# Windowed attention inside a two-layer feed-forward kernel: the probabilities of the loop are normalised and turned by VectorE in 32x32 blocks instead of by TensorE, the heads are turned straight out of PSUM, and the values run three steps after their scores

## What is computed

```python
scores = scale * np.matmul(q_c, k_full.transpose(0, 1, 3, 2))      # 32 queries x 64 keys
scores = scores - np.max(scores, axis=-1, keepdims=True)
a = np.exp(scores)
a = a / (np.sum(a, axis=-1, keepdims=True) + 1e-09)
out[:, :, c_start:c_end] = np.matmul(a, v_full)
...
h = x @ w_in;  g = np.maximum(0.01 * h, h);  x = g @ w_out          # first block, 512 -> 2048 -> 512
...
h = x @ w_in2; g = P(h) / (Q(h) + 1e-6);     y = g @ w_out2         # second block, the same sizes
```

## Time and profile before

| | |
|---|---|
| median of 3 runs | 1153.5 us (1151.1 to 1154.75) |
| profiled execution, its own time | 1152.93 us |
| its span in the trace | 1151.1 us |
| PE busy | 1136.9 us, 99% |
| VectorE busy | 741.6 us, 64% |
| ScalarE busy | 565.9 us, 49% |
| GpSimd busy | 132.6 us, 12% |
| granted TensorE clock, mean | 0.997 of full speed |

### The profile page before, as it was taken

How to read it: one execution, slowest core, us unless ns; L and a number is a source line. 1 busy time by engine, 2 the same in 40 slices (tenths; PEclk the granted TensorE clock), 3 DMA queues, 4 the chain that set the end, 5 groups by cost and what they waited for, 6 DMA issues and landing times.

```text
span 1151.1 us, 22841 instructions
## 1 busy us (share of the span) xinstructions
PE 1136.9 (99%) x8950; PEld 1066.0 (93%) x8950; DVE 741.6 (64%) x1385; ACT 565.9 (49%) x1184; POOL 132.6 (12%) x132
## 2 busy tenths in 40 slices
PE   7999999999999999999999999999999999999998
PEld 6999999999999999999999999999999999999996
DVE  5554444444445454443327888888888888888886
ACT  4223223323233332322227676676767667676765
POOL 4991120211202112100000000000000000000000
PEclk8999999999999999999999999999999999999999
DMA  7662434334434255210786010020201002020000
GB/s 265 198 201 102 169 108 156 130 114 157 163 131 154 74 184 175 83 56 2 285 278 241 1 65 18 1 83 1 83 1 71 13 1 83 1 83 1 28 1 28
DMA packets 44311, 114.77 MB, mean 100 GB/s; under 512 B 5040, under 2 KB 5168, under 8 KB 44208
## 3 DMA queue, kind: packets, MB, share of 16 engines
q1 hardware_dynamic: 44208, 113.33, 28.5%
HBM read 77.66 MB, written 35.65 MB: 98 GB/s over the span
## 4 chain that ended last, share of the span: by engine, by line
PE 95%; DVE 2%; ACT 1%; issue 1%; DMA 0%; SPq 0%; DVEq 0%
PE psum L512 15%; PE psum L514 15%; PE psum L513 15%; PE psum L527 8%; PE psum L546 8%; PE psum L547 8%; PE psum L545 8%; PE psum L528 7%; PE psum L529 7%; PE psum L484 2%; PE psum L461 1%; PE psum L469 1%; DVE g_lo L860 1%; DVE scratch L857 0%; ACT g_hi L688 0%
## 5 line engine op out<-in xcount | busy, mean ns | idle before, releaser
L512 PE MATMUL psum<-x_hi,w_hi 128*128 128x384 f32 x1020 | 342.5, 336 | 1.5 <-DVE x_lo L851 1.5
L514 PE MATMUL psum<-x_hi,w_lo 128*128 128x384 f32 x1020 | 342.6, 336 | 0.0
L513 PE MATMUL psum<-x_lo,w_hi 128*128 128x384 f32 x1020 | 341.6, 335 | 0.0
L857 DVE TENSOR_TENSOR scratch<-psum,scratch 128x384 f32<-128x384 f32 x128 | 71.3, 557 | 237.6 <-ACT scratch L682 236.9
L682 ACT ACTIVATE scratch<-psum 128x384 f32<-128x384 f32 x128 | 62.8, 491 | 279.2 <-PE psum L514 275.3
L512 PEld LDWEIGHTS psum<-x_hi,w_hi 128*128 128x128 f32 x1020 | 191.5, 188 | 8.4 <-issue 2.3
L513 PEld LDWEIGHTS psum<-x_lo,w_hi 128*128 128x128 f32 x1020 | 191.5, 188 | 5.4
L514 PEld LDWEIGHTS psum<-x_hi,w_lo 128*128 128x128 f32 x1020 | 191.4, 188 | 0.0
L527 PE MATMUL psum<-g_hi,w_hi 128*128 128x384 f32 x512 | 177.5, 347 | 0.0
L529 PE MATMUL psum<-g_hi,w_lo 128*128 128x384 f32 x512 | 171.3, 335 | 0.0
L528 PE MATMUL psum<-g_lo,w_hi 128*128 128x384 f32 x512 | 171.2, 334 | 0.0
(11 more groups left out here) (75 smaller groups left out, 1407.4 us busy)
## 6 DMA issues: line engine op xcount, KB each, us to landing
raw<-weights_in SPq DMA_DIRECT2D x64, 256.0 KB, 4.1
scratch<-groups_in SPq DMA_DIRECT2D x21, 768.0 KB, 6.1
scratch<-groups_in SPq DMA_DIRECT2D x21, 512.0 KB, 4.4
w_hi_scratch<-w_high SPq DMA_DIRECT2D x32, 256.0 KB, 4.1
w_lo_scratch<-raw SPq DMA_DIRECT2D x32, 256.0 KB, 4.5
w_hi<-w_hi_scratch SPq DMA_DIRECT2D x32, 256.0 KB, 3.6
w_lo<-w_lo_scratch SPq DMA_DIRECT2D x32, 256.0 KB, 4.5
x_hi_scratch<-x_hi SPq DMA_DIRECT2D x8, 768.0 KB, 3.3
```

The source lines that it names most:

```text
L512: nc.tensor.matmul(bank, hi, x_hi[:, b, k, :], start=(k == 0), stop=False)
L513: nc.tensor.matmul(bank, hi, x_lo[:, b, k, :], start=False, stop=False)
L514: last = nc.tensor.matmul(bank, lo, x_hi[:, b, k, :], start=False, stop=(k == KT - 1))
```

## The change

Only the 21 groups inside the loop change; the first three keep the old functions under new names (`scores_first`, `values_first`, `save_first_heads`, and `first_maxima` with the exponential `first_exp`, which two of them had already).

In the loop the subtraction of the maximum goes into the bias of the exponential, which becomes eight activations of 64 columns, each with its row sum as a second output. DVE then inverts the sums, multiplies all probabilities by them, and turns them with eight transposes, each on 32 partitions by 256 columns. PE's four transposes, ACT's copy and DVE's sum of the rows go. The products of the values run after `gemm1` of the third step after their scores, not the second; DVE turns their result from PSUM directly and saves it in that same step. PE waits with the next scores for `turned`, no longer for `x_ready`. The order of the 32 products within the scores and within the values changes too, and with it the layout of `q`, `k` and `v` in the input, of the same size.

```diff
-TRANSPOSE_AT = {f + 1: g for f, g in SCORES_AT.items()}
-VALUES_AT = {f + 2: g for f, g in SCORES_AT.items()}
-SAVE_AT = {f + 3: g for f, g in SCORES_AT.items()}
+TURN_AT = {f + 1: g for f, g in SCORES_AT.items()}
+VALUES_AT = {f + 3: g for f, g in SCORES_AT.items()}
...
                 if not own_place:
-                    pe.wait_ge(x_ready, g)
+                    pe.wait_ge(turned, g)
...
             def scores(c, at):
+
+                for cc in range(CPG):
+                    for u in range(2):
+                        for q in range(SLOTS):
+                            st, j = q // 2, 2 * u + q % 2
+                            last = nc.tensor.matmul(
+                                psum[CHUNK * q:CHUNK * (q + 1), at.bank + u, KEYS * cc:KEYS * (cc + 1)],
+                                q_of(ring(c), st, j, cc), k_of(ring(c), st, j, cc), start=True, stop=True)
...
+                if own_place:
+                    pe.wait_ge(probs_t_ready, g + 1)
+                else:
+                    pe.wait_ge(probs_turned, g - GPT + 1)
 
             def values(c, at):
+
+                for cc in range(CPG):
+                    for j in range(SLOTS):
+                        for st in range(SETS):
+                            q0 = (j % 2) * 2 * P + (j // 2 * CPG + cc) * CHUNK
+                            last = nc.tensor.matmul(
+                                at.loop_values_at[CHUNK * j:CHUNK * (j + 1), st, :, cc, :],
+                                at.probs_t[DH * st:DH * (st + 1), q0:q0 + CHUNK],
+                                v_of(ring(c), st, j, cc), start=True, stop=True)
...
-                        if f in TRANSPOSE_AT:
-                            transpose_probs(g0 + TRANSPOSE_AT[f], loop_att[TRANSPOSE_AT[f]])
...
+            def loop_exp(g, at):
+
+                act.wait_ge(shifted, g + 1)
+                for u in range(2):
+                    for c in range(CPG):
+                        n = CPG * u + c
+                        last = nc.scalar.activation(at.loop_probs[:, n, :], at.scores[:, u, c, :], ACT.Exp,
+                                                    scale=SCALE, bias=at.safe[:, n:n + 1],
+                                                    accum_out=at.loop_sums[:, n:n + 1])
+                last.then_inc(exp_ready, 1)
...
+            def turn_probs(g, at):
+
+                dve.wait_ge(exp_ready, g + 1)
+                nc.vector.tensor_scalar(at.safe, at.loop_sums, SUM_EPS, None, ALU.add).then_inc(sums_ready, 2)
+                dve.wait_ge(sums_ready, 3 * g + 2)
+                nc.vector.reciprocal(at.loop_inv, at.safe).then_inc(sums_ready, 1)
+                dve.wait_ge(sums_ready, 3 * g + 3)
+                nc.vector.tensor_tensor(at.loop_probs, at.loop_probs,
+                                        at.loop_inv.unsqueeze(2).broadcast_to([P, SETS * CPG, KEYS]),
+                                        ALU.mult).then_inc(normalised, 1)
+                dve.wait_ge(normalised, g + 1)
+                for q in range(SLOTS):
+                    for h in range(2):
+                        to = CHUNK * (q // 2 * 2 + h)
+                        last = nc.vector.transpose(
+                            at.probs_t[to:to + CHUNK, (q % 2) * 2 * P:(q % 2 + 1) * 2 * P].rearrange("p (n k) -> p n k", k=CHUNK),
+                            at.loop_halves[CHUNK * q:CHUNK * (q + 1), :, h, :])
+                last.then_inc(probs_turned, 1)
+
+            def turn_values(g, at):
+
+                dve.wait_ge(heads_ready, g + 1)
+                nc.vector.transpose(at.probs_t.rearrange("p (s n) -> p s n", s=SETS), at.loop_values).then_inc(turned, 1)
```

More of the change, by code:

```diff
@@ L161, in build @@
     probs_t_ready = S("probs_t_ready")
+    probs_turned = S("probs_turned")
     heads_ready = S("heads_ready")
@@ L224, in __init__ @@
             self.heads_tv = probs_t.rearrange("p (e k n) -> p e k n", e=2, k=KT)
+            self.loop_probs = probs.rearrange("p (n k) -> p n k", k=KEYS)
+            self.loop_halves = probs.rearrange("p (n h k) -> p n h k", h=2, k=CHUNK)
+            self.loop_values = psum[:, bank:bank + 2, 0:2 * SETS * DH]
+            self.loop_values_at = self.loop_values.rearrange("p s (h c r) -> p s h c r", h=DHALVES, r=CHUNK)
+            self.loop_heads = probs_t.rearrange("p (k n) -> p k n", k=KT)
+            self.loop_sums = st[:, 1, :]
+            self.loop_inv = st[:, 3, :]
             self.max_v = st[:, 0, :].rearrange("p (s c) -> p s c", s=SETS)
@@ L486, in values @@
                                     at.probs_t[DH * c2:DH * (c2 + 1), q0:q0 + CHUNK],
-                                    v_of(ring(c), st, j, cp, c2), start=True, stop=True)
+                                    first_v_of(ring(c), st, j, cp, c2), start=True, stop=True)
                 last.then_inc(heads_ready, 1)
@@ L613, in first_scores @@
                 wait_scores(g, g, own_place=True)
-                scores(g, first_att[g])
+                scores_first(g, first_att[g])
             def first_values(g):
-                wait_values(g, g)
-                values(g, first_att[g])
+                wait_values(g, g, own_place=True)
+                values_first(g, first_att[g])
             pe.wait_ge(zeros_ready, 1)
@@ L669, in save_probs_t, with save_heads, save_first_heads @@
                 nc.scalar.copy(at.probs_t, psum[:, at.bank, :]).then_inc(probs_t_ready, 1)
-            def save_heads(g, gi, b, at, t=None):
+            def save_heads(g, gi, b, at, t):
                 act.wait_ge(turned, g + 1)
-                if t is not None and gi == 0:
+                if gi == 0:
                     act.wait_ge(y_stored, 32 * t + 1)
+                nc.scalar.copy(x_hi[:, b, :, P * gi:P * (gi + 1)], at.loop_heads).then_inc(xh_ready, 1)
+            def save_first_heads(g, gi, b, at):
+                act.wait_ge(turned, g + 1)
                 to = x_hi[:, b, :, P * gi:P * (gi + 1)].rearrange("p k (e n) -> p e k n", e=2)
@@ L742, in tile_a @@
                         if f in SCORES_AT:
[L743 to L747, removed]
+                            loop_exp(g0 + SCORES_AT[f], loop_att[SCORES_AT[f]])
+                        if f in VALUES_AT:
+                            save_heads(g0 + VALUES_AT[f], VALUES_AT[f], (tp + 1) % 2, loop_att[VALUES_AT[f]], t)
                 save_y_high(t, tp)
@@ L813, in first_maxima, with loop_maxima, save_low @@
                 nc.vector.tensor_scalar(at.safe, at.st[:, 0, :], -SCALE, None, ALU.mult).then_inc(shifted, 1)
+            def loop_maxima(g, gi, tp, t, at):
+                dve.wait_ge(scores_ready, g + 1)
+                edge = None
+                if tp == 0 and gi == 0:
+                    edge = at.scores[:, :, 0, N_MEM:N_MEM + LEFT]
+                if tp == 1 and gi == GPT - 1:
+                    edge = at.scores[:, :, CPG - 1, KEYS - RIGHT:KEYS]
+                if edge is not None:
+                    nc.vector.tensor_scalar(edge, edge, NEG, None, ALU.add).then_inc(masked, 1)
+                    dve.wait_ge(masked, t + 1)
+                first_maxima(g, at)
+            def turn_probs(g, at):
[18 more added lines that the diff above has]
+                nc.vector.transpose(at.probs_t.rearrange("p (s n) -> p s n", s=SETS), at.loop_values).then_inc(turned, 1)
+            def save_low(g, gi, b, at):
+                dve.wait_ge(xh_ready, g + 1)
+                cols = slice(P * gi, P * (gi + 1))
+                nc.vector.tensor_tensor(x_lo[:, b, :, cols], at.loop_heads, x_hi[:, b, :, cols].bitcast(F32),
+                                        ALU.subtract).then_inc(x_ready, 1)
             def first_inverses(g, at):
@@ L1002, in windows @@
         return full.reshape(BATCH, HEADS, n_groups, CPG, KEYS, DH)
-    slots = np.array([[SLOTS * (p // 2) + 2 * (p % 2) + (r + p // 2) % 2 for r in range(2)] for p in range(HEADS // 2)])
+    slots = np.array([[SLOTS * (p // 2) + 2 * ((r + p // 2) % 2) + p % 2 for r in range(2)] for p in range(HEADS // 2)])
     qg = q.reshape(BATCH, HEADS, n_groups, P, DH)[:, slots].transpose(0, 3, 2, 5, 1, 4)
     kg = windows(k, mem_k)[:, slots].transpose(0, 3, 2, 6, 1, 4, 5)
-    vg = windows(v, mem_v).reshape(BATCH, SETS, SLOTS, n_groups, 2, 2, KEYS, DH).transpose(0, 3, 4, 6, 1, 5, 2, 7)
+    vw = windows(v, mem_v).reshape(BATCH, SETS, SLOTS, n_groups, CPG, KEYS, DH)
+    vg = vw.transpose(0, 3, 1, 5, 4, 2, 6).reshape(GROUPS, P, -1)
+    first_vg = vw.reshape(BATCH, SETS, SLOTS, n_groups, 2, 2, KEYS, DH).transpose(0, 3, 4, 6, 1, 5, 2, 7).reshape(GROUPS, P, -1)
+    vg = np.concatenate([first_vg[:GPT], vg[GPT:]])
     groups = np.concatenate([a.reshape(GROUPS, P, -1) for a in (qg, kg, vg)], axis=2)
```

36 lines of the change are left out of this document (20 added, 16 removed).

## The result

The changed kernel takes 1156.39 us (median of 20 runs, 1154.13 to 1159.04) against 1152.94 for the kernel before (20 runs): ratio 1.0032, 95% interval 1.0024 to 1.0041. The forecast was 1145.3 us with a range from 1141 to 1156. It was wrong, and in its sign. The profiled execution of the changed kernel has a span of 1153.6 us where the one before had 1151.1. Of the later experiments, one run of e1 (3978.97 us) and one of e3 (1840.88 us) were slow ones, and their ratios go without them.

A forecast was written before the change was run, and what follows sets the result against it. TensorE, busy 99% of the span, was taken to bound the kernel. Removing 13.1 us of transposes and waits, less 3.4 and 1.5 us of POOL stalls, gave 8.2 us gain: 1145.3 us, range 1141 to 1156.

The forecast's parts named there:

- What goes: On PE: 21 groups' transposes (9.3 us), their waits for the exponential (1.6) and for x_lo (2.2) disappear, 13.1 us together.
- the waits for `x_lo`: PE before the scores: three stalls from DVE's late x_lo, 2.2 us together, vanish because PE waits for turned instead.
- the sum: PE time removed by the change: 9.3 + 1.6 + 2.2 = 13.1 us, before stalls are taken off.
- What moves at no cost: PE's products of scores and values: new order taken as free, 0.99 us each; a price could make 4 us either way.
- SP's delay of one step: SP's load of v and the weights' stores and loads come one step later, with 61 us of cover.
- The new chain: On DVE and ACT, from H (end of the gemm1 before the maxima): probs_turned at 193.75, 0.1 us before PE's deadline.
- The choice between 2.9 and 3.8 us for the turning: DVE's eight transposes per group: 2.9 us if they overlap (rival, chance 0.24), 3.8 us if not; the upper taken.
- The spare: Between the end of the DVE and ACT chain and PE's deadline before the values: 0.1 us left.
- POOL's surcharge: PE stalls from DVE instructions reading two SBUF tiles beside POOL: 3.4 us in the first tile, 1.5 us later.
- The dear transposes: Rival: DVE's transposes cost more, PE waits for probs_turned in all 21 groups; 1165.9 us at 0.60 each; slower, chance 0.13.
- in most groups: Sign that the forecast is wrong: PE stands before the values in most groups.
- The forecast's own number: Whole kernel: 13.1 - 3.4 - 1.5 = 8.2 us faster, 1145.3 us; chance 0.40.

The follow-up runs named there:

- e1: Changed kernel with the loop groups' row maxima in PSUM, read there by the scaling: 1150.28 us, 0.9984 of the kernel before.
- e3: Changed kernel with POOL's splits of the second block's weights cut to 8 of 512 columns: 1151.09 us, 0.9990 of the kernel before.
- e10: Kernel before without the loop's transposes on PE and ACT's copy behind them: 1141.66 against 1153.17 us, 0.9903.
- e7: e2 with the hidden tile also kept in PSUM: 1140.52 us, 0.9882 of the kernel before; second go 1142.32 us, 0.9908.
- e9: Kernel before with only the hidden tile kept in PSUM between the maximum and g_lo: 1150.71 against 1153.17 us, 0.9982.
- e5: Changed kernel with neighbouring DVE transposes on the same 32 partitions, one execution: the eight take 3.09 us in place of 3.59.
- e2: e1 with epsilon's output and the inverses also in PSUM: 1143.3 against 1151.63 us for the kernel before, 0.9930.
- c0: Changed kernel again with no edit, on a second chip: 1157.38 against 1153.32 us for the kernel before, 1.0038.
- e8: e1 without adding epsilon, the reciprocal made directly from the sums: 1145.55 us, 0.9924 of the kernel before.

## Why the prediction was wrong

**What goes** was right. The transposes and their waits were put at 10.9 us, and e10 measured 11.2 us (9.2 to 13.0). With the waits for `x_lo` the sum was 13.1 us; e7, in which no stall is left before the values, gains 13.6 and 10.6 us in two goes. It removes the same waits for the exponential and for `x_lo` as e9, so the two gains don't add. No wait for `x_lo` before the scores stands in the trace after.

**What moves at no cost** was right. Scores and values still take 0.99 us each in their new order, and SP's delay of one step cost nothing visible.

**The new chain** was right: H + 12.36 measured for H + 12.47. The choice between 2.9 and 3.8 us for the turning fell on the right side, measured 3.59, and e5 shows why the upper one holds. The spare was 0.3 us rather than 0.1.

**The step that failed is POOL's surcharge.** It was put at 3.4 + 1.5 = 4.9 us and measured 13.8 us of stalls (8.3 + 5.5), with 1.6 us at the lower clock behind them. Its list had three instructions that wait for POOL, those that read two tiles from SBUF. It left out the two small ones that the change puts into the chain, the scaling of the maxima (L865) and the epsilon (L883). They read one tile and write eight columns, I priced them at 0.17 us, and each takes up to 1.25 us when POOL is at work. For the later groups I looked at `g_lo` alone and found it at the edges of POOL's work; L865 starts 1.2 us after it, between these edges, and met POOL in seven groups. There it made the 5.5 us, as e1 and e3 show from both sides. In the first tile it is four or five waits in a row. By their durations less the undisturbed ones, L865 waited 2.3 us in the three groups, L883 2.6, `g_lo` 2.1 and the multiplication 1.1. So the three instructions that I had priced waited 3.2 us, about the 3.4 that I gave them (after the spare), and the two that I had left out waited 4.9 us; together they made stalls of 8.3 us.

The kernel before had the warning in it. Its own small instruction on such columns, L828, has a median of 172 ns and a longest of 548, by the source view of that line:

```profile
L828 DVE TENSOR_SCALAR stats<-stats x22: 170/172/548, 10.2 to 524.1; 128x8 f32<-128x8 f32 x22
```

I had taken its duration from a clean group. The Trainium skill states the mechanism too (SBUF — State Buffer, Who interferes with whom): `tensor_scalar` may use the port pair that DVE shares with POOL, which is held by one of them for a whole instruction, and `tensor_reduce` never does. The runs agree: `tensor_scalar` took 1.24 us beside POOL from SBUF and 0.166 always from PSUM (e1), and the `tensor_reduce` of the kernel before that reads SBUF (L826) took at most 0.682 us, beside POOL too. No transpose in the 168 of the changed kernel was over 0.442 us either.

**The clock** was in no term. After a stall of 3.9 us in the first group PE ran 3.4 us at half its clock and lost 1.6 us more.

**Of the rivals** none named what happened. The dear transposes had the right wait and the wrong cause; that PE stands before the values "in most groups" did not come true either (10 of 21). The gain was there; it was given back to a wait of an instruction that I had counted as nothing.

**Luck.** The forecast's own number, 8.2 us faster, is near what e2 measures, 8.1 us, but by chance: e2 takes the multiplication out of POOL's way as well and has 2.0 us of stalls left where the forecast had 4.9, so the sum would give it 11.1. The traces show where the rest went. Ahead of the loop the granted clock is at half for a time that differs from one execution to the next (6.8 us in the kernel before and in the changed kernel, 13.7 in c0's execution of the same kernel and in e2's), and the loop's first scores start at 30.39 us in the kernel before and at 31.94 in e2. Counted from these scores to the end, the kernel before takes 1120.7 us, the changed kernel 1123.2 (2.5 more, the sum says 2.3), e2 1109.6 (11.1 less), and e7 1107.0 and 1107.2 in its two goes (13.7 and 13.5 less, the sum says 13.1). With 1.6 us lost ahead of the loop, and a kernel before that is 1.3 us faster on e2's chip than its profiled execution, e2's 8.1 comes out. What sets the time at the lower clock ahead of the loop is open.

Open is how the first tile's loss divides among the two small instructions, the multiplication and `g_lo`. The durations say how long each waited in this execution, not what its absence would save: each wait moves the next one against POOL's rhythm, as e1 and e8 show, so the shares don't add.

## What to carry to other kernels

When an instruction is added to a chain with little to spare, look at the longest duration of its kind in the trace and not only at the mean of a clean stretch, and ask what made it long. The size of a VectorE instruction says nothing on its wait for GpSimd: here eight columns waited as long as 512. A spare of a few tenths of a microsecond on the path that sets the end should be priced as a stall wherever another engine's instruction of a microsecond can fall into it; keeping small operands in PSUM took the wait away here.

## What the hardware showed that I had not expected

- An eight-column scaling of VectorE from SBUF to SBUF took 1.24 us beside GpSimd and 0.17 without; from PSUM it took 0.165 to 0.167 us in all 21 places.
- Being let go by GpSimd puts VectorE just behind the start of GpSimd's next instruction: the multiplication after such a wait took 1.61 to 1.63 us in the three groups of e1's first tile, and 0.87 in those of e8.
- A stall of PE of 3.9 us was followed by the granted clock at half for 3.4 us; those of 1.7 and 2.6 us in the same trace were not. The length of the stall alone doesn't settle it: of e5's three, 2.5, 2.6 and 2.5 us long, the last was followed by 3.4 us at half the clock and the others were not.
